# Reading a per-tile flag from a table instead of computing it in registers, in the expert stage of an attention and mixture-of-experts kernel

## The chip, the cores and the metric

The kernel runs on one core of a Trainium2 chip. The metric is the device time of one execution in microseconds (us), lower is better. Engines are named as the profile names them: PE (TensorE), ACT (ScalarE), DVE (VectorE), POOL (GpSimd), SP (SyncE, which here only issues DMAs). Each engine has a sequencer that reads its instruction stream; the profile marks what the sequencer does by itself (register arithmetic, branches, semaphore waits, register loads) with a q, as in ACTq.

## The reference

Three layers follow each other: windowed attention with sink keys (4 x 8 heads, 768 positions, head size 64), a mixture of experts over 3072 tokens, and a dense layer pair.

```python
def _moe_ref(x, w_skip, w_gate, w1, w2):            # x: 3072 x 512, 8 experts, F = 1024
    out = x.copy()
    do_compute = (x @ w_skip) > 0                     # the other tokens pass through
    xc = x[do_compute]
    e_idx = np.argmax(xc @ w_gate, axis=1)            # one expert for each token
    for e in range(8):
        h = np.maximum(xc[e_idx == e] @ w1[e], 0.0)
        y[e_idx == e] = gate_w[e_idx == e, None] * (h @ w2[e])
    out[do_compute] = xc + y
    return out

def _moe2_ref(x, w_in, w_out):                        # 512 -> 2048 -> 512
    r = np.maximum(x @ w_in, 0.0)
    return (r * r) @ w_out
```

## The kernel before, in words

The three layers run one after the other; the change touches the second, the expert stage, which takes the span's part from about 195 to 391 us. Tokens have been sorted by expert into rows of `routed`. The stage walks over tiles of 128 tokens, numbered n = 0, 1, 2 ..., and every expert e owns the tiles from `first` to `end`. How many an expert has is known only while the kernel runs: DVE computes it into the SBUF row `table`, and each engine reads `first` and `end` of an expert into registers with two `value_load` calls (lines 381 and 382). In this data there are 15 tiles: expert 0 has n = 0 to 2, experts 1 to 4 have two each (3 and 4, 5 and 6, 7 and 8, 9 and 10), experts 5 and 6 have one each (11 and 12), expert 7 has 13 and 14. The bodies for experts 0 and 1 are written out; experts 2 to 7 run in a hardware loop (line 373) whose body holds two experts, and inside each body a loop over n runs the tile's code.

Matrix products are made of an upper and a lower part of each operand for accuracy. While PE works on expert e with one pair of weight buffers, the next expert's weights are split into the other pair: SP loads them as 8 chunks of 512 KB into `w_raw`, ACT copies each chunk to `w_hi` (1.04 us or so), DVE subtracts to `w_lo` (1.22 us), and then SP may load the chunk of the expert after that into the same place. The eight chunks are two groups, the head (4 chunks, before the tile's own work) and the tail (4 chunks, in its middle). This is done in an expert's first tile. In later tiles of the same expert the same code makes one chunk of each group again, so that all counts of semaphores stay simple. The number that tells these apart is the flag `later`: 0 in the first tile of an expert, 1 in later ones. ACT and DVE need it in every tile (number of chunks, first chunk, values to wait for), ACT needs it a second time for the tile before, and SP needs it once per expert, for the expert's last tile.

Before, the flag is register arithmetic, `min(max(n - first, 0), 1)`:

```python
ahead, more, flag = (eng.alloc_register(...) for _ in range(3))
eng.reg_alu(ahead, n, first, op=ALU.subtract)
eng.reg_alu(more, ahead, 0, op=ALU.max)
eng.reg_alu(flag, more, 1, op=ALU.min)
```

Within a tile, ACT's order is: head chunks (line 748), `relu_b` for half 0 of the hidden layer (tile `h_b`, line 710), `hb_hi` (714), `relu_b` for half 1, `xb_hi` of the next tile (673), `hb_hi` again, tail chunks (748). PE's order is: layer 1 (line 975) for half 0 and the first half of half 1, then `turn_h(0)`, a transpose of ACT's `h_b` (line 983), the rest of layer 1, the transpose of the next tile's tokens (967), and layer 2 (994). DVE's order is: head chunks (1430), `hb_lo` (1385), `xb_lo` (1306), `hb_lo`, tail chunks, and the output row `y_row` and `y_id` (1392, 1394). All engines work through their streams in order.

Of the kernel before, what the change touches and what calls it, by code (L numbers as in the profile page):

```python
# [22 lines left out]
F32, F32R, BF16, I32 = mybir.dt.float32, mybir.dt.float32r, mybir.dt.bfloat16, mybir.dt.int32  # L23
# [17 lines left out]
MAX_TILES = N // P + 2 * E  # L41
# [3 lines left out]
UNIT = 8  # L45
HEAD = 4
# [27 lines left out]
def build(nc, n_sink, window, qT, kT, v, v_sink, w_route, weights, out):  # L74
# [10 lines left out]
    with ctx:  # L85
        def sem(name):
            return ctx.enter_context(nc.semaphore(name))
# [33 lines left out]
        def sbr(name, shape, dt):  # L121
            return sb(name, shape, dt, small, "right")

        pad_row = sbr("pad_row", [P, ROW], F32)
        table = sbr("table", [1, 3 * E], I32)
        rows = sbr("rows", [1, MAX_TILES + 2], I32)
        least = sbr("least", [1, E], F32)
        tile_no = sbr("tile_no", [1, MAX_TILES + 2, E], I32)
        row_of = sbr("row_of", [1, 4, MAX_TILES + 2, E], F32)
# [82 lines left out]
        s_xstore = [sem(f"s_xstore{n}") for n in range(XR)]  # L212
        s_scatter = [sem(f"s_scatter{n}") for n in range(XR)]
        s_tchain, s_table, s_padrow = sem("s_tchain"), sem("s_table"), sem("s_padrow")
        s_rchain, s_rows = sem("s_rchain"), sem("s_rows")

        s_w0 = [sem(f"s_w0{n}") for n in range(UNIT)]
        s_whead, s_wtail = sem("s_whead"), sem("s_wtail")
# [128 lines left out]
            first, size = ((0, HEAD), (HEAD, UNIT - HEAD))[k]  # L347
            return size - later * (size - 1), later * (size - 1) + first

        def is_later(eng, n, first):  # L350

            ahead, more, flag = (eng.alloc_register(f"later_{nc.next_id()}") for _ in range(3))
            eng.reg_alu(ahead, n, first, op=ALU.subtract)
            eng.reg_alu(more, ahead, 0, op=ALU.max)
            eng.reg_alu(flag, more, 1, op=ALU.min)
            return nc.s_assert_within(eng.snap(flag), 0, 1, skip_runtime_bounds_check_because="held to 0 and 1 above")

        def chunk_at(k, shift):

# [8 lines left out]
        def each_expert(eng, body):  # L368

            for e in range(2):  # L370
                first, end = expert_tiles(eng, e)
                body(e, e, 0 if e == 0 else first, end)
            with eng.Fori(1, E // 2) as m:
                for slot in range(2):
                    e = m * 2 + slot
                    first, end = expert_tiles(eng, e)
                    body(e, slot, first, end)
# [9 lines left out]
        def _(eng):  # L387
# [85 lines left out]
            def expert(e, slot, first, end):  # L473

                made = parts_ahead(e, first)
                for f in range(UNIT):
                    if f == HEAD - 1 or f == UNIT - 1:
                        last = parts_ahead(e + 1, end) - (UNIT - HEAD if f < HEAD else 0)
                        if f < HEAD:
                            last = is_later(eng, end - 1, first) * (UNIT - HEAD - 1) + last  # L480
                        eng.wait_ge(s_wlo, last)
                        close(eng)
                    else:
                        eng.wait_ge(s_wlo, made + f + 1)
                        close(eng)
                    load_chunk(e + 2, f)
# [137 lines left out]
        def _(eng):  # L624
# [105 lines left out]

            def tile(e, n, slot, first):

                later = is_later(eng, n, first)

                def chunks(k):
                    size, shift = group(k, later)
                    made = parts_ahead(e, n) + (later * (UNIT - 2) if k == 0 else later * (UNIT - HEAD - 1) + HEAD)
                    eng.wait_ge(s_whi, made)
                    close(eng)

                    before_is_later = is_later(eng, n, first + 1) if k == 0 else 0
                    lower = parts_ahead(e, n) + later * (UNIT - 2)
                    eng.wait_ge(s_wlo, lower if k == 1 else lower - (UNIT - HEAD) + before_is_later * (UNIT - HEAD - 1))
                    close(eng)
                    chunk_loaded(e + 1, k * HEAD)
                    with eng.Fori(0, size) as c:
                        f = bass.ds(chunk_at(c, shift), 1)
                        eng.activation(w_hi[1 - slot][:, f, :], w_raw[:, f, :], ACT.Copy).then_inc(s_whi, 1)  # L748

                chunks(0)  # L750
                relu_b(n, 0)
                h_upper(n, 0)
                relu_b(n, 1)
                x_upper(n + 1)
                h_upper(n, 1)

                eng.wait_ge(s_by, n + 1)
                chunks(1)
# [6 lines left out]
            gate(TILES - 1)  # L765
            first_tile()
            eng.wait_ge(s_table, 1)
            each_expert(eng, expert)


# [366 lines left out]
        def _(eng):  # L1137
# [266 lines left out]
            chain(eng.scalar_tensor_tensor(out=row_of[:, 3, :, :], in0=row_of[:, 0, :, :], scalar=0.0, in1=row_of[:, 2, :, :], op0=ALU.is_ge, op1=ALU.mult))  # L1404
            chain.end()
            eng.tensor_reduce(rows[:, :], row_of[:, 3, :, :], AX.X, ALU.max).then_inc(s_rows, 1)
            h_lower(0, 0)
            h_lower(0, 1)
            for f in range(0, 3):
# [4 lines left out]
            for f in range(4, UNIT):  # L1414
                lower_chunk(eng, 1, f, (s_whi, UNIT + f + 1), s_wlo)
            eng.wait_ge(s_table, 1)

            def tile(e, n, slot, first):
                later = is_later(eng, n, first)

                def chunks(k):
                    size, shift = group(k, later)
# [15 lines left out]

            def expert(e, slot, first, end):
                with eng.Fori(1 if isinstance(e, int) and e == 0 else first, end) as n:  # L1440
                    tile(e, n, slot, first)
            each_expert(eng, expert)


# [86 lines left out]
```

## Time and profile before

| | |
|---|---|
| median of three runs | 961.18 us (961.46, 955.9, 961.18) |
| the profiled execution's own time | 961.46 us |
| span of the profile, first to last instruction | 960.0 us |
| mean granted TensorE clock | 0.989 of full speed |
| PE busy | 928.3 us, 97% of the span |
| DVE, ACT busy | 456.0 and 419.8 us |
| PE waits inside the expert stage that are laid to ACT's `h_b` | 3.9 us, 3 times |

The span and the time differ by 1.46 us in the profiled execution, for what lies around the first and last instruction. The busy time of ACT and DVE counts only their data instructions; what a sequencer does by itself does not count, so an engine that shows as idle can have a busy sequencer.

### The profile page before, as it was taken

The page shows a single profiled execution, that of the slowest core. Times are in us where ns is not written, and L with a number is a line of the kernel's source. Part 1 is how long each engine was busy: PE and PEld are TensorE (multiplying, and loading weights), DVE is VectorE, ACT ScalarE, POOL GpSimd, SP SyncE. Part 2 cuts the span into 40 slices and gives each one's busy share as a digit, 9 for nine tenths or more (in the row PEclk, how much of TensorE's full clock was granted, in tenths as well). Part 3 has the DMA queues.
Part 4 walks back from the last instruction along what each step waited for, and adds up shares of the span by engine and source line. Part 5 has one row for each costly group of instructions (what it writes and reads, how often), then busy time and mean ns, then how long its engine had stood idle before and what let it go on. Part 6 is the DMA issues. An engine that isn't in the chain of part 4 may idle for free.

```text
span 960.0 us, 17066 instructions
## 1 busy us (share of the span) xinstructions
PE 928.3 (97%) x5240; PEld 743.9 (77%) x5241; DVE 456.0 (47%) x1392; ACT 419.8 (44%) x969; POOL 82.4 (9%) x148
## 2 busy tenths in 40 slices
PE   7999999989999999599999999999999999999998
PEld 5778777767888877488888888888888888888886
DVE  5787899785767778343232223222322222222223
ACT  6888999745666677243122123112321222122122
POOL 3112111223111111000000000000000000000000
PEclk9999999989999999799999999999999999999999
DMA  5456774376666687600020002000200020002001
GB/s 179 167 169 207 226 233 149 121 278 215 240 238 223 224 314 256 240 4 1 0 71 19 1 1 87 0 0 0 87 0 0 0 87 0 0 0 87 0 0 44
DMA packets 40291, 100.04 MB, mean 104 GB/s; under 512 B 5821, under 2 KB 5949, under 8 KB 40240
## 3 DMA queue, kind: packets, MB, share of 16 engines
q1 hardware_dynamic: 33936, 83.33, 25.5%
q0 software_dynamic: 6160, 16.02, 4.8%
q8 instruction: 25, 0.41, 0.2%
q14 instruction: 26, 0.21, 0.1%
q10 hardware_dynamic: 144, 0.07, 0.0%
HBM read 78.25 MB, written 25.56 MB: 108 GB/s over the span
## 4 chain that ended last, share of the span: by engine, by line
PE 90%; DVE 3%; DMA 2%; issue 2%; ACT 1%; DVEq 0%; ACTq 0%; SPq 0%; POOLq 0%; POOL 0%
PE bank L1090 28%; PE bank L1104 28%; PE bank L994 7%; PE bank L975 7%; PE bank L834 5%; PE bank L889 4%; PE bank L862 4%; PE bank L900 1%; PE bank L983 1%; DMA w_raw<-in_weights 1%; PE bank L1071 1%; PE bank L914 1%; PE bank L882 1%; PE bank L967 1%; ACT prob L640 0%
## 5 line engine op out<-in xcount | busy, mean ns | idle before, releaser
L1455 DVE TENSOR_TENSOR g<-relu_c 128x512 f32<-128x512 f32 x96 | 66.5, 692 | 364.9 <-ACT relu_c L780 364.8
L780 ACT ACTIVATE relu_c<-bank 128x512 f32<-128x512 f32 x96 | 57.4, 598 | 388.6 <-PE bank L1090 388.6
L1090 PE MATMUL bank<-x_hi,w_lo 128*128 128x512 f32 x384 | 152.6, 398 | 0.8 <-DVE x_lo L1448 0.8
L1104 PE MATMUL bank<-w_hi,g_lo 128*128 128x512 f32 x384 | 153.1, 399 | 0.0
L1090 PE MATMUL bank<-x_lo,w_hi 128*128 128x512 f32 x384 | 152.8, 398 | 0.0
L1090 PE MATMUL bank<-x_hi,w_hi 128*128 128x512 f32 x384 | 152.8, 398 | 0.0
L1104 PE MATMUL bank<-w_hi,g_hi 128*128 128x512 f32 x384 | 152.0, 396 | 0.0
L1104 PE MATMUL bank<-w_lo,g_hi 128*128 128x512 f32 x384 | 151.8, 395 | 0.0
L640 ACT ACTIVATE prob<-score,neg_max 128x264 f32<-128x264 f32 (+1 forms) x192 | 94.0, 496 | 16.6 <-DVE neg_max L1164 16.6
L1430 DVE TENSOR_TENSOR w_lo<-w_raw,w_hi x70 | 82.0, 1221 | 21.2 <-ACT w_hi L748 11.1
L1090 PEld LDWEIGHTS bank<-x_hi,w_lo 128*128 128x128 f32 x384 | 72.6, 189 | 19.0 <-DVE x_lo L1448 1.2
L1090 PEld LDWEIGHTS bank<-x_lo,w_hi 128*128 128x128 f32 x384 | 72.7, 189 | 17.9
L1090 PEld LDWEIGHTS bank<-x_hi,w_hi 128*128 128x128 f32 x384 | 72.8, 190 | 17.5
L1104 PEld LDWEIGHTS bank<-w_hi,g_hi 128*128 128x128 f32 x384 | 72.3, 188 | 17.6
L1104 PEld LDWEIGHTS bank<-w_lo,g_hi 128*128 128x128 f32 x384 | 72.4, 188 | 16.9
L1104 PEld LDWEIGHTS bank<-w_hi,g_lo 128*128 128x128 f32 x384 | 72.1, 188 | 16.8
L1164 DVE CUSTOM_DVE_ANT_0 score<-bank,masks 128x264 f32<-128x264 f32 (+1 forms) x192 | 74.5, 403 | 16.0 <-PE bank L834 7.3
L748 ACT ACTIVATE w_hi<-w_raw x70 | 69.5, 1051 | 18.5 <-DVE w_lo L1430 9.5
L1459 DVE TENSOR_TENSOR g_lo<-g,g_hi 128x512 fp32r<-128x512 f32 x96 | 65.8, 686 | 7.7 <-ACT g_hi L786 7.7
L786 ACT ACTIVATE g_hi<-g 128x512 fp32r<-128x512 f32 x96 | 59.9, 624 | 9.9 <-PE bank L1104 9.9
L834 PE MATMUL bank<-k_in,q_in 64*128 64x264 f32 (+1 forms) x384 | 55.9, 409 | 5.7 <-DMA k_in<-in_kT 5.6
L862 PE MATMUL bank<-ident,prob 128*128 128x128 f32 x352 | 56.1, 283 | 3.6 <-ACT probT L653 2.9
(141 smaller groups left out, 1285.3 us busy)
## 6 DMA issues: line engine op xcount, KB each, us to landing
w_raw<-in_weights SPq DMA_DIRECT2D x80, 512.0 KB, 5.1
x_c<-x_rows SPq DMA_DIRECT2D x28, 256.0 KB, 3.6
k_in<-in_kT SPq DMA_DIRECT2D x24, 264.0 KB
q_in<-in_qT SPq DMA_DIRECT2D x24, 256.0 KB, 3.1
v_in<-in_v SPq DMA_DIRECT2D x24, 256.0 KB
x_rows<-x_row SPq DMA_DIRECT2D x24, 256.0 KB
out<-w_raw SPq DMA_DIRECT2D x12, 512.0 KB, 2.8
x_res<-routed POOLq DMA_DIRECT2D x16, 260.0 KB, 4.5
```

The source lines that it names most:

```text
L640: eng.activation(prob[:, i % 2, h, 0:width(i)], score[:, i % 2, h, 0:width(i)], ACT.Exp, bias=neg_max[:, i % 2, h:h + 1], scale=-1.0, accu ...
L748: eng.activation(w_hi[1 - slot][:, f, :], w_raw[:, f, :], ACT.Copy).then_inc(s_whi, 1)
L834: eng.matmul(score_ps[n % SCORE_BANKS][:, 0:width(i)], q_in[rows, i % 3, h // 2, :], keys, start=True, stop=True).then_inc(s_score, 1)
L862: ins = eng.transpose(to[:, u * P:(u + 1) * P], prob[:, i % 2, 2 * k + half, at * KB + NS:(at + 1) * KB], ident[:, :])
L975: ins = eng.matmul(h_ps[half][:, :], x[:, c, :], w[:, c, cols], start=(c == 0 and k == 0), stop=(c == DC - 1 and k == 2))
L994: ins = eng.matmul(y_ps[:, :], h[:, c // 4, at], w[:, DC + c // 2, cols], start=(c == 0 and k == 0), stop=(c == FC - 1 and k == 2))
L1090: ins = eng.matmul(hc_ps[f % 2][:, :], w[f // UNIT][:, f % UNIT, wcols], x[:, c, :], start=(c == 0 and n == 0), stop=(c == DC - 1 and n == 2))
L1104: ins = eng.matmul(yc_ps[s][:, :], gg[:, f % 2, s * P:(s + 1) * P], w[f // UNIT][:, f % UNIT, DM:CH], start=(f == 0 and n == 0), stop=(f = ...
L1164: eng.tensor_tensor_reduce(score[:, i % 2, h, 0:width(i)], score_ps[n % SCORE_BANKS][:, 0:width(i)], masks[:, mask_kind(i), 0:len(blocks(i ...
L1430: eng.tensor_tensor(w_lo[1 - slot][:, f, :], w_raw[:, f, :], w_hi[1 - slot][:, f, :].bitcast(F32), ALU.subtract).then_inc(s_wlo, 1)
L1455: eng.tensor_tensor(g[:, f % 2, :], relu_c[:, f % 2, :], relu_c[:, f % 2, :], ALU.mult).then_inc(s_cg, 1)
L1459: eng.tensor_tensor(g_lo[:, f % 2, :], g[:, f % 2, :], g_hi[:, f % 2, :].bitcast(F32), ALU.subtract).then_inc(s_cglo, 1)
```

## The change

The flag of every tile is computed once, by DVE, right behind the row numbers `rows`: a compare of `row_of[:, 0]` (tile number less the first tile of each expert) with zero, and a minimum over the experts, into the new SBUF row `later_tile`, with a semaphore `s_later`. `is_later` then is a `value_load` from that row at index n. ACT and DVE wait for `s_later` once, before their loops; SP before its first use of it in experts 0 and 1. For the tile before, ACT reads index n - 1. That value is 1 at the first tile of an expert if the expert before had more than one tile, where the arithmetic gave 0, so the number that ACT waits for on `s_wlo` there is higher by 3.

```diff
+        later_tile = sbr("later_tile", [1, MAX_TILES + 2], I32)
...
-        def is_later(eng, n, first):
-
-            ahead, more, flag = (eng.alloc_register(f"later_{nc.next_id()}") for _ in range(3))
-            eng.reg_alu(ahead, n, first, op=ALU.subtract)
-            eng.reg_alu(more, ahead, 0, op=ALU.max)
-            eng.reg_alu(flag, more, 1, op=ALU.min)
-            return nc.s_assert_within(eng.snap(flag), 0, 1, skip_runtime_bounds_check_because="held to 0 and 1 above")
+        def is_later(eng, n):
+
+            return eng.value_load(later_tile[0:1, bass.ds(n, 1)], min_val=0, max_val=1)
...
                         if f < HEAD:
-                            last = is_later(eng, end - 1, first) * (UNIT - HEAD - 1) + last
+                            if isinstance(e, int):
+                                eng.wait_ge(s_later, 1)
+                            last = is_later(eng, end - 1) * (UNIT - HEAD - 1) + last
...
-                later = is_later(eng, n, first)
+                later = is_later(eng, n)
...
-                    before_is_later = is_later(eng, n, first + 1) if k == 0 else 0
+                    before_is_later = is_later(eng, nc.s_assert_within(n - 1, 0, MAX_TILES, skip_runtime_bounds_check_because="tile 0 is written out")) if k == 0 else 0
...
             eng.tensor_reduce(rows[:, :], row_of[:, 3, :, :], AX.X, ALU.max).then_inc(s_rows, 1)
+            eng.tensor_scalar(row_of[:, 1, :, :], row_of[:, 0, :, :], 0.0, None, ALU.not_equal).then_inc(s_rchain, 1)
+            eng.wait_ge(s_rchain, 6)
+            eng.tensor_reduce(later_tile[:, :], row_of[:, 1, :, :], AX.X, ALU.min).then_inc(s_later, 1)
```

The first place is ACT at the start of a tile, in the looped body for experts 3, 5 and 7, from the entry of the loop over n to the first head chunk. Before (an ISA row is one fused group of register operations, or an assertion behind a load):

```order
L738 ISA
L353 ISA [waits s_whi]
L743 REGISTER_ALU
L310 ISA [waits s_wlo]
L746 UNCONDITIONAL_BRANCH [waits s_whead]
L746 ISA
L748 ACTIVATE w_hi<-w_raw 128x1024
```

The same place after the change:

```order
L353 TENSOR_LOAD later_tile
L353 ISA x2
L737 ISA
L353 ISA [waits s_whi]
L353 TENSOR_LOAD later_tile
L353 ISA x2
L742 ISA
L311 ISA [waits s_wlo]
L745 UNCONDITIONAL_BRANCH [waits s_whead]
L745 ISA
L747 ACTIVATE w_hi<-w_raw 128x1024
```

Two loads, each with its two ISA rows, stand between the loop's entry and the first chunk; the second is behind the wait for `s_whi`, ACT's own last chunk.

The second place is DVE at the start of a tile, in the same body. Before:

```order
L1440 UNCONDITIONAL_BRANCH
L1440 ISA
L1424 ISA
L1426 UNCONDITIONAL_BRANCH [waits s_wlo]
L1426 ISA
L1430 ISA [waits s_whi]
L1430 REGISTER_ALU
L1430 TENSOR_TENSOR w_lo<-w_raw,w_hi 128x1024
```

After:

```order
L1445 UNCONDITIONAL_BRANCH
L1445 ISA
L353 TENSOR_LOAD later_tile
L353 ISA x2
L1429 ISA
L1431 UNCONDITIONAL_BRANCH [waits s_wlo]
L1431 ISA
L1435 ISA [waits s_whi]
L1435 REGISTER_ALU
L1435 TENSOR_TENSOR w_lo<-w_raw,w_hi 128x1024
```

One load comes in ahead of DVE's first chunk of each tile. Once in the kernel, two DVE instructions come in ahead of `hb_lo` of tile 0:

```order
L1406 TENSOR_REDUCE rows<-row_of 1x42 [waits s_rchain]
L1407 TENSOR_SCALAR row_of<-row_of 1x336
L1409 TENSOR_REDUCE later_tile<-row_of 1x42 [waits s_rchain]
L1385 TENSOR_TENSOR hb_lo<-bank,hb_hi 128x512 [waits s_bhhi] x2
L339 TENSOR_TENSOR w_lo<-w_raw,w_hi 128x1024 [waits s_whi] x3
L1306 TENSOR_TENSOR xb_lo<-bank,xb_hi 128x512 [waits s_bxhi]
```

The new instructions are rows two and three; everything below them on DVE's stream stands two places later than before.

## Rows read from the trace of the kernel before

**Rows 1.** The page: busy time of each engine.

```profile
PE 928.3 (97%) x5240; PEld 743.9 (77%) x5241; DVE 456.0 (47%) x1392; ACT 419.8 (44%) x969; POOL 82.4 (9%) x148
```

**Rows 2.** Busy time by stretch: PE, PEld, DVE, ACT, POOL, granted clock, DMA share, GB/s.

```profile
213.00:391.30 178.30, 173.94 (x840) 141.12 (x840) 124.56 (x146) 111.15 (x143) 34.82 (x48) 1.00 0.71 250
```

**Rows 3.** Waits of PE, 195 to 392 us: total us, times, longest.

```profile
PE bank L983 <- ACT h_b L710: 3.9, 3, 1.8
...
PE bank L975 <- DVE xb_lo L1306: 0.5, 1, 0.5
```

**Rows 4.** Timeline of PE: start, us, instruction [idle before, releaser]; transposes of `h_b`.

```profile
217.77 0.44 PE L983 MATMUL bank<-ident,h_b 128*128 128x128 f32 x2 [0.42 <-ACT h_b L710]
...
316.54 0.60 PE L983 MATMUL bank<-ident,h_b 128*128 128x128 f32 x4
...
341.21 0.60 PE L983 MATMUL bank<-ident,h_b 128*128 128x128 f32 x4
...
355.86 0.66 PE L983 MATMUL bank<-ident,h_b 128*128 128x128 f32 x4 [1.73 <-ACT h_b L710]
```

**Rows 5.** Timeline of ACT at first tiles of an expert.

```profile
315.50 0.57 ACT L710 ACTIVATE h_b<-bank 128x512 f32<-128x512 f32 x1
...
333.23 1.06 ACT L748 ACTIVATE w_hi<-w_raw  x1
336.13 3.90 ACT L748 ACTIVATE w_hi<-w_raw  x4 [1.85 <-DVE w_lo L1430]
340.05 0.60 ACT L710 ACTIVATE h_b<-bank 128x512 f32<-128x512 f32 x1
...
351.42 3.90 ACT L748 ACTIVATE w_hi<-w_raw  x4 [1.92 <-DMA w_raw<-in_weights]
355.23 0.57 ACT L710 ACTIVATE h_b<-bank 128x512 f32<-128x512 f32 x1
```

**Rows 6.** Waits of ACT, 213 to 392 us: total us, times, longest.

```profile
ACT h_b L710 <- PE bank L975: 20.0, 20, 3.9
ACT w_hi L748 <- DVE w_lo L1430: 9.5, 5, 2.1
```

**Rows 7.** Chain that ended last, ACT's and DVE's sequencers around 348 and 351 us.

```profile
347.79 0.28 ACTq L381
...
348.44 0.28 ACTq L382
...
351.08 0.31 DVEq L381
...
351.73 0.07 DVEq L382
```

**Rows 8.** Single lines on the sequencers: duration ns min/median/max, first and last start.

```profile
L353 ACTq FUSED_REGOPS  x14: 175/178/181, 215.6 to 378.7; - x14
L761 ACTq FUSED_REGOPS  x14: 172/192/198, 212.5 to 376.6; - x14
L1440 DVEq FUSED_REGOPS  x14: 207/242/253, 218.0 to 379.7; - x14
L381 DVEq TENSOR_LOAD <-table x8: 314/322/1092, 215.5 to 365.4; - x8
```

**Rows 9.** Timeline of DVE: rows for the row numbers, `xb_lo`, and a head group.

```profile
206.77 0.49 DVE L1406 TENSOR_REDUCE rows<-row_of 1x42 int32<-1x336 f32 x1
...
211.79 0.67 DVE L1306 TENSOR_TENSOR xb_lo<-bank,xb_hi 128x512 fp32r<-128x512 f32 x1
...
340.61 2.36 DVE L1430 TENSOR_TENSOR w_lo<-w_raw,w_hi  x2 [2.29 <-issue]
```

**Rows 10.** Timeline of SP: the first reload of a head chunk at tile 11.

```profile
342.08 0.33 SPq L415 DMA_DIRECT2D w_raw<-in_weights  x1
```

**Rows 11.** Busy time by stretch, as in Rows 2, around tiles 11 and 12.

```profile
340.00:342.00 2.00, 2.00 (x13) 1.67 (x12) 1.39 (x2) 0.79 (x3) 0.81 (x2) 1.00 0.39 110
...
358.00:360.00 2.00, 2.00 (x14) 1.70 (x12) 1.63 (x3) 1.29 (x3) 0.55 (x1) 1.00 0.89 320
```

More of the change, by code:

```diff
@@ L214, in build @@
         s_tchain, s_table, s_padrow = sem("s_tchain"), sem("s_table"), sem("s_padrow")
-        s_rchain, s_rows = sem("s_rchain"), sem("s_rows")
+        s_rchain, s_rows, s_later = sem("s_rchain"), sem("s_rows"), sem("s_later")
         s_w0 = [sem(f"s_w0{n}") for n in range(UNIT)]
@@ L767, in _ @@
             eng.wait_ge(s_table, 1)
+            eng.wait_ge(s_later, 1)
             each_expert(eng, expert)
@@ L1416, in _, with tile @@
             eng.wait_ge(s_table, 1)
-            def tile(e, n, slot, first):
-                later = is_later(eng, n, first)
+            eng.wait_ge(s_later, 1)
+            def tile(e, n, slot):
+                later = is_later(eng, n)
                 def chunks(k):
@@ L1440, in expert @@
                 with eng.Fori(1 if isinstance(e, int) and e == 0 else first, end) as n:
-                    tile(e, n, slot, first)
+                    tile(e, n, slot)
             each_expert(eng, expert)
```

## The prediction

> **What bounds the kernel now.** I read the page first: PE is busy for 97% of the span [rows 1], so a change to register code on other engines costs something only where PE waits for one of them. The change touches the expert stage alone, so the next views are that stage's. From the start of tile 1 to the end of tile 14 PE is busy for 173.94 of 178.30 us at a granted clock of 1.00, which is the 2.4 GHz level [rows 2]. Its waits from 195 us on are few, and the largest kind is the transpose of `h_b` waiting for ACT: three times, 3.9 us in all, the longest 1.8 us [rows 3]. They stand in tiles 1, 12 and 13: 0.42 us at 217.77, 1.73 us at 355.86, and the 1.8 us of the third [rows 3, 4]. These three tiles are already late, and what makes ACT or its weights later there is paid in full.
>
> The first tiles of experts 1 to 5 (n = 3, 5, 7, 9 and 11) show no wait, so the question is how much room they have. At n = 11 ACT makes the four head chunks from 336.13 and runs straight into `h_b` at 340.05, which ends at 340.65; PE takes it at 341.21 [rows 4, 5]. Where PE was waiting, it began 0.06 us after `h_b` ended (355.23 + 0.57 against 355.86 [rows 4, 5]). So the room at n = 11 is 341.21 - 340.65 - 0.06 = 0.50 us. At n = 9 it is 316.54 - 316.07 - 0.06 = 0.41 us [rows 4, 5]; n = 3, 5 and 7 repeat n = 11's pattern with 0.51 us each. **This is the figure the case turns on: a delay of ACT's head group under half a microsecond is free, and all above it is PE's.**
>
> What starts that head group is the next thing to read. At n = 11 the chunk before it starts at 333.23 and the group at 336.13, 2.90 us later, of which ACT's data path is idle for 1.85 us. The view names DVE's `w_lo` as releaser [rows 5], but the count that ACT waits for there had been reached a tile earlier; the gap comes at all five of these tiles, 9.5 us in all, 2.1 at most [rows 6], because it is the sequencer's own work: the end of one loop, two loads from `table`, the flag, the waits, the next loop. One chunk of 1.06 us does not cover that. Instructions added to the sequencer there are therefore exposed.
>
> **Price of one load.** The loads of lines 381 and 382 are of the same form as the new ones: one number from an SBUF row, its bounds check and assertion. On ACT the first starts at 347.79 and the second, with its address in front of it, at 348.44: 0.65 us each with the address [rows 7]. On DVE the load with its check takes 351.73 - 351.08 = 0.65 us [rows 7], and some 0.11 us more with its address: 0.76 us.
>
> **ACT, per tile.** Two loads come in, 2 x 0.65 = 1.30 us. The second flag's fused group of 0.18 us (L353) goes, and the group at the loop's entry that held the first flag (0.19 us, L761) becomes the first load's address, which is in the 0.65 already [rows 8]. Net x = 1.30 - 0.18 - 0.19 = 0.93, say **0.9 us**. From below x is bounded by two bare loads of 0.28 us less the two groups, 0.2 us, and from above by nothing saved: 1.3 us [rows 7, 8]. I take 0.9 because it is built of the same instructions on the same sequencer. By tile:
> - n = 3, 5, 7: 0.9 - 0.51 = 0.39 us each, 1.2 us. n = 9: 0.9 - 0.41 = 0.5 us.
> - n = 1: the sequencer runs ahead of four queued chunks, so the first load is hidden behind them; the second stands behind the wait for ACT's last chunk. It adds 0.65 - 0.18 = 0.5 us to an `h_b` for which PE already waits (0.42 us [rows 4]): 0.5 us.
> - n = 2 and second tiles (4, 6, 8, 10, 14): only one chunk is made, and `h_b` then waits for PE; these are among the 20 waits of 20.0 us in all, 1.0 us each on average [rows 6]. The first load hides behind the tail chunks, the second's 0.5 us fits into that wait. Nothing.
> - n = 12, 13: ACT waits for the DMA of the weights (1.92 us at 351.42 [rows 5]), and the loads fit into that wait. What moves the DMA is DVE.
>
> **DVE, per tile.** One load comes in, 0.76 us, and the fused group at the loop's entry (0.24 us, L1440 [rows 8]) shrinks to the address: net some **0.5 us**, between 0.1 (the bare load of 0.32 less that group) and 0.8 us. In two-tile experts DVE has room: nothing on PE waits for it but the 0.5 us at the stage's start [rows 3]. It matters where SP's reloads feed the next tile, n = 11 to 13. There the head group starts when the sequencer is ready (340.61, 2.29 us idle, released by issue [rows 9]). SP issues the first reload at 342.08 [rows 10], and at that time the DMA engines are at 39% [rows 11], so a reload issued 0.5 us later lands 0.5 us later; this weight's arrival ends ACT's wait at 351.42 and so PE's at 355.86. I charge 0.5 us at n = 12, which takes in n = 11's own 0.4. At n = 13 DVE is later by its own load once more, but by then the DMA engines are at 89% and more [rows 11] and the chunks queue behind each other, so I charge nothing there, at most 0.5 us. Together **0.5 us, at most 1.2.**
>
> **DVE, once.** Two instructions of the size of the reduce at 206.77, 0.49 us each with 336 elements [rows 9], come in: 1.0 us. `xb_lo` for tile 1 then ends at 213.5 instead of 212.46 [rows 9], and PE, which comes to it at 213.00, waits up to 0.5 us. It is not lost a second time: PE waits for `h_b` at 217.77 in the same tile, and by n = 1's line above that wait ends at 218.27 whether PE comes early or late. Cover: that wait, 0.42 + 0.5 us. Without it the cost would be 0.5 us. POOL's `s_rows` comes before the new pair and does not move.
>
> **SP and the raised count.** SP's load is done before it waits for DVE's last chunk. In two-tile experts that wait lasts most of a tile. At n = 11 and 12 the load stands between the third and the fourth reload, 1.2 us apart [rows 9], and may make the fourth 0.2 us late, behind a full queue: nothing. The wait for `s_wlo` that is higher by 3 asks for DVE's head chunk of the tile before, which is done long before ACT comes there: nothing.
>
> **Sum.** 0.5 (n = 1) + 1.2 (n = 3, 5, 7) + 0.5 (n = 9) + 0.5 (n = 11 to 13) = **2.7 us**. The profiled execution took 961.46 us, so it would be 964.2; the median of the runs shown is 0.28 us below that, so I predict 963.9, rounded to **964.0 us**, 0.3% slower. The last layer, from 403 us on, reads no flag and has the same instructions.
>
> **The rivals.**
> - *All hidden, 961.5 us.* The sequencer reads a load while the engine works on queued instructions, as at 347.79, amid tile 11's tail chunks [rows 7]. If that held everywhere, only n = 1's half microsecond or less would be left. Against it: at n = 3 to 11 one chunk of 1.06 us covers a path of 2.90 us [rows 5]. For it: x could be near its lower end, 0.2 us, and under 0.5 us five of the terms are zero. The Trainium skill (Advanced Engine Details and Errata, Sequencer and Instruction Queues with Engine Queue Depths) says that other engine instructions are queued while a control instruction executes and gives ScalarE and VectorE a queue of 8; by that alone all loads would be hidden. The trace agrees with it at 347.79 and not at 336.13, where the queue had run dry.
> - *Slower on the other side of 1%, 974 us.* The first load on DVE took 1.09 us, against a median of 0.32 [rows 8]. If reading a row that another engine wrote cost every load 0.8 us more, x would be 2.5 us: five tiles with 2.0 each, n = 1 with 1.3, and 1.3 for n = 11 to 13, 12.6 us in all. It decides from x above 2.0. Against it: seven of eight loads were near the median, and the slow one was the first behind a new wait.
> - *Moved code, 968.5 us.* ACT's program grows by 26 instructions and DVE's by 15, so code in the looped body sits elsewhere in memory. If each of the three passes through it then had to fetch instructions again, at 1.5 us each (a gap of the size ACT's sequencer already hides or shows at 336.13 [rows 5]), 4.5 us would come on top. Nothing in the trace speaks for it. The Trainium skill (the same page, ISA Cache) gives a cache of two lines of 256 instructions outside TensorE; no row here shows a refetch.
> - *The flags save time, 959 us.* The removed register work is 0.37 us per ACT tile; even free loads would give back at most that at n = 1 and some tenths at 12 and 13, under 1.5 us. No path to 1%.
>
> **How the numbers follow.** Likeliest (962.5 to 966) 0.64; all hidden (961 to 962.5) 0.18; moved code or loads somewhat dearer than priced (966 to 970.5) 0.12; over 970.8 us 0.04; saving 0.02. A measurement of this kernel tells about 1% (9.6 us) from no change: faster by more than that 0.01, within it 0.95, slower 0.04. The costs alone would give 961 to 968.5. One of the three runs shown is 5.3 us below the others, and a median could fall there, which takes the low end to 957.5. Range 957.5 to 968.5.
>
> **What would show it.** In the changed profile: ACT's head group starts 3.8 instead of 2.90 us after the chunk before it at n = 3 to 11; waits of PE for `h_b` of about 0.4 us appear there, five new ones beside the three old; the wait at tile 1 grows to 0.9 us; loads of line 353 take 0.28 us on ACT and 0.32 on DVE. The prediction is wrong if those head groups start no later, or if loads are far from 0.3 us, or if the difference lies outside 213 to 391 us.

## The result, and the profile after

The kernel after takes 963.03 us (median of 15 runs, 960.11 to 968.17), the kernel before, run beside it, 958.64 us (15 runs, 954.69 to 961.76). The ratio is 1.0058 with a 95% interval of 1.0038 to 1.0079, so the change costs 5.6 us, between 3.6 and 7.6: slower, and within the 1% that the prediction called no change. (The ratio is worked out from the single times and is not the quotient of the two medians, which lie 4.4 us apart; the means lie 5.6 apart. The same holds for the ratios below.) Its profiled execution took 963.35 us. All ratios are of fast runs; one run of the kernel before, of 29 in the first set below, took 1824.7 us and is in none of them.

The page after (PE's busy time is 1.3 us longer than in [rows 1]), the windows, and the waits of PE from 195 to 392 us:

```profile
PE 929.6 (97%) x5240; PEld 742.6 (77%) x5241; DVE 456.8 (47%) x1394; ACT 418.9 (44%) x969; POOL 82.2 (9%) x148
```

```profile
213.00:356.00 143.00, 140.53 (x666) 111.45 (x664) 95.04 (x112) 86.09 (x112) 27.88 (x38) 1.00 0.68 236
356.00:361.00 5.00, 4.42 (x17) 3.65 (x18) 3.62 (x4) 1.91 (x5) 0.00 (x0) 0.66 0.96 343
```

```profile
PE bank L983 <- ACT h_b L709: 4.2, 4, 2.0
PE bank L967 <- DMA x_raw<-routed: 1.2, 1, 1.2
PE bank L975 <- DVE xb_lo L1306: 0.8, 1, 0.8
```

Two things stand out against [rows 2, 3]. PE's waits for `h_b` have hardly grown (4.2 us in 4 waits, before 3.9 in 3), although five new ones were forecast. And in the second window the granted clock is 0.66, where before it was 1.00.

The delay on ACT is there, to the tenth. ACT's timeline after, tile 11, which answers to 333.23 to 340.05 in [rows 5], and the load itself:

```profile
333.09 1.06 ACT L747 ACTIVATE w_hi<-w_raw  x1
336.88 3.90 ACT L747 ACTIVATE w_hi<-w_raw  x4 [2.73 <-issue]
340.69 0.57 ACT L709 ACTIVATE h_b<-bank 128x512 f32<-128x512 f32 x1
```

```profile
L353 ACTq TENSOR_LOAD <-later_tile x28: 273/278/640, 208.8 to 380.9; - x28
...
L353 DVEq TENSOR_LOAD <-later_tile x14: 298/313/808, 214.6 to 381.9; - x14
```

The head group starts 3.79 us after the chunk before it, instead of 2.90. But PE is not ready for `h_b` when it was. The transposes of `h_b` at n = 3, 4, 9, 11 and 12 (`turn_h(0)`), as in [rows 4]:

```profile
240.03 0.66 PE L983 MATMUL bank<-ident,h_b 128*128 128x128 f32 x4
...
252.63 0.60 PE L983 MATMUL bank<-ident,h_b 128*128 128x128 f32 x4
...
316.11 0.66 PE L983 MATMUL bank<-ident,h_b 128*128 128x128 f32 x4 [0.27 <-ACT h_b L709]
...
341.32 0.66 PE L983 MATMUL bank<-ident,h_b 128*128 128x128 f32 x4
...
356.58 1.04 PE L983 MATMUL bank<-ident,h_b 128*128 128x128 f32 x4 [1.99 <-ACT h_b L709]
...
361.42 0.60 PE L983 MATMUL bank<-ident,h_b 128*128 128x128 f32 x4
```

The last row is `turn_h(1)` of n = 12. In the kernel before it is this row, behind the `turn_h(0)` at 355.86 in [rows 4]:

```profile
359.10 0.60 PE L983 MATMUL bank<-ident,h_b 128*128 128x128 f32 x4
```

From n = 3 to n = 4, where nothing is waited for, PE takes 252.63 - 240.03 = 12.60 us. Before it took 12.32. PE's program is the same, so its matmuls themselves must follow each other more slowly. The starts of layer 1's matmuls show it. (The distance from one start to the next is called the pitch below.) Ahead of `turn_h(0)` stand 18 of them; tile 6 in the kernel before:

```profile
275.40 0.39 PE L975 MATMUL bank<-w_lo,xb_hi 128*128 128x512 f32 x1
...
279.26 0.39 PE L975 MATMUL bank<-w_hi,xb_hi 128*128 128x512 f32 x1
279.49 0.38 PE L983 MATMUL bank<-ident,h_b 128*128 128x128 f32 x2
```

and after:

```profile
273.72 0.39 PE L975 MATMUL bank<-w_lo,xb_hi 128*128 128x512 f32 x1
...
277.68 0.40 PE L975 MATMUL bank<-w_hi,xb_hi 128*128 128x512 f32 x1
277.92 0.60 PE L983 MATMUL bank<-ident,h_b 128*128 128x128 f32 x4
```

(279.49 - 275.40) / 18 = 227 ns from start to start, against (277.92 - 273.72) / 18 = 233 ns. Before, some half of each tile ran at 227 ns and the rest, behind the transposes, at 231 to 236; after, all of it runs at 233. The timeline's durations hardly show this (0.39 and 0.40), and no wait does; starts do. So do mean durations of many like instructions, if one compares them closely: the matmuls `bank<-w_hi,xb_lo` from 213 to 345 us take 390 ns on average before and 395 after. The last layer ran at 233.6 ns in both.

So three things had to be explained: the slower pitch, the loads, and tile 12, where `turn_h(1)` came 4.84 us behind `turn_h(0)` instead of 3.24.

The two profiled executions differ by only 1.9 us in span (961.9 and 960.0). From `turn_h(0)` of tile 0 to that of tile 14 the one after takes 185.79 us, the one before 179.87: 5.92 more. But the stretch ahead of it is 3.66 us shorter (199.12 against 202.78 us) and the one behind it 0.37. The new loads have no part in the stretch ahead: the first starts at 208.8 us. From 195 to 213 us the granted clock was 0.83 before and 0.96 after.

### The profile page after: what moved, and what is told of

Same layout as the page of the kernel before. It is cut to its first block, busy times and chain, and to the rows that moved or that the text cites. A ratio compares the mean times of both kernels' runs of the same rounds, so it can differ in the third digit from the quotient of the medians.

```text
span 961.9 us, 17222 instructions
## 1 busy us (share of the span) xinstructions
PE 929.6 (97%) x5240; PEld 742.6 (77%) x5241; DVE 456.8 (47%) x1394; ACT 418.9 (44%) x969; POOL 82.2 (9%) x148
## 4 chain that ended last, share of the span: by engine, by line
PE 89%; issue 3%; DMA 2%; ACT 2%; DVE 2%; ACTq 1%; DVEq 0%; SPq 0%; POOLq 0%; POOL 0%
PE bank L1090 28%; PE bank L1104 28%; PE bank L994 7%; PE bank L975 6%; PE bank L834 5%; PE bank L889 4%; PE bank L862 4%; PE bank L983 1%; PE bank L900 1%; PE bank L1071 1%; PE bank L914 1%; PE bank L882 1%; PE bank L967 1%; DMA w_raw<-in_weights 1%; ACT w_hi L747 1%
## 5 line engine op out<-in xcount | busy, mean ns | idle before, releaser
L747 ACT ACTIVATE w_hi<-w_raw x70 | 69.5, 1050 | 27.4 <-issue 15.6
```

## The experiments

### First set: where the slower pitch comes from

The new row `later_tile` stands in the middle of a group of SBUF tiles that are laid out downwards. Each tile declared behind it moves down by 192 bytes, `xb_hi`, `xb_lo`, `h_b`, `hb_hi` and `hb_lo` among them, from a multiple of 128 bytes to 64 past one. The first kernel has the move alone:

```diff
         rows = sbr("rows", [1, MAX_TILES + 2], I32)
+        unused = sbr("unused", [1, MAX_TILES + 2], I32)
```

> The kernel before, with nothing changed but an unused row of 168 bytes declared where the change declares later_tile. No instruction is added; the tiles declared behind it (xb_hi, xb_lo, h_b, hb_hi, hb_lo, y_row) lie 192 bytes lower, so that their start is no longer a multiple of 128 bytes. Theory A (the place of TensorE's stationary operands sets the pitch of its matmuls): the matmuls of 512 columns in the expert stage follow each other at 233 ns as after the change, not at 227 to 232, and the time is 3 to 3.5 us over before. Theory B (the slower pitch comes with the new loads or the moved code of ACT and DVE): pitch as before, difference 0. Theory C (the pitch is a matter of the single execution): it follows neither.

Measured: ratio 1.0029 (1.0011 to 1.0047), 2.8 us slower, from a row that nothing reads. Tile 6 in its trace:

```profile
273.20 0.39 PE L976 MATMUL bank<-w_lo,xb_hi 128*128 128x512 f32 x1
...
277.17 0.40 PE L976 MATMUL bank<-w_hi,xb_hi 128*128 128x512 f32 x1
277.41 0.60 PE L984 MATMUL bank<-ident,h_b 128*128 128x128 f32 x4
```

(277.41 - 273.20) / 18 = 234 ns. From n = 2 to n = 11 this trace loses 1.83 us against before, 0.20 in each tile, with no wait added. Theory A holds, and B and C fall. Its 3 to 3.5 us were a little high, but inside the interval of 1.1 to 4.5. The edit moves every tile declared behind it, those of ACT and DVE too; which of them matter is a question for the last set.

The second kernel has the change, with the row where it moves nothing:

```diff
-        later_tile = sbr("later_tile", [1, MAX_TILES + 2], I32)
...
         y_id = sbr("y_id", [P, 1], I32)
+        later_tile = sbr("later_tile", [1, MAX_TILES + 2], I32)
```

> The whole change, with later_tile declared last of its group, so that no other tile moves. Theory A: the pitch is that of before, ACT's head groups still start 3.8 us after the chunk before them, so PE now waits for h_b some 0.3 us at n = 3, 5, 7 and 11 and 0.6 us at n = 9, and n = 12 costs 0.6 us: about 2.5 us over before, less than the 5.6 us of the change. Theory B: 5 to 6 us over before and a pitch of 233 ns.

Measured: 1.0019 (1.0005 to 1.0033), 1.8 us over before (0.5 to 3.2), where 2.5 were expected. The pitch is 227 ns again, and now the waits that the prediction foresaw are there. ACT's and PE's timelines at n = 9:

```profile
307.11 1.06 ACT L747 ACTIVATE w_hi<-w_raw  x1
311.27 3.90 ACT L747 ACTIVATE w_hi<-w_raw  x4 [3.10 <-issue]
315.08 0.57 ACT L709 ACTIVATE h_b<-bank 128x512 f32<-128x512 f32 x1
```

```profile
315.70 0.66 PE L983 MATMUL bank<-ident,h_b 128*128 128x128 f32 x4 [0.48 <-ACT h_b L709]
```

`h_b` ends at 315.65 and PE takes it 0.05 us later. The intervals from one `turn_h(0)` to the next at n = 3, 5, 7, 9 and 11 are 12.65, 12.70, 12.60, 12.94 and 12.58 us, where before they were 12.36 each. At n = 12 the interval is 15.67 instead of 14.64 (0.6 more was expected), and at n = 13, where the granted clock fell as in the kernel after, 15.72 instead of 14.38.

The third keeps the row in place and adds 64 bytes, for a move of 256:

```diff
         later_tile = sbr("later_tile", [1, MAX_TILES + 2], I32)
+        unused = sbr("unused", [1, 16], I32)
```

> The whole change, with 64 unused bytes behind later_tile, so that the tiles behind lie 256 bytes lower and again begin at a multiple of 128 bytes. Theory A with 128 bytes as the step: pitch and time as with later_tile declared last, about 2.5 us over before. Theory A with another step, or some neighbour that matters: 233 ns and 5 to 6 us over before. Theory B: 5 to 6 us.

Measured: 1.0028 (1.0012 to 1.0044), 2.7 us over before, with the pitch of before (227.9 ns over layer 1 from 240 to 345 us, against 228.1 before and 233.0 after). So it is the position against 128 bytes, not the move, that counts. Its intervals at n = 3 to 11 repeat those of the second kernel to 0.03 us. The times of these two and of the kernel with the move alone can't be told from each other (1.8, 2.7 and 2.8 us, each known to 1.3 to 1.7); it is the pitches and the intervals that tell the causes apart.

If that is so elsewhere too, the last layer of the kernel before has something to give: `x_hi`, `x_lo`, `g_hi` and `g_lo` begin 96 bytes past a multiple of 128. The expectation calls all four moving operands, that is, operands whose 512 columns are streamed past a stationary one of 128x128. That is right for `x_hi` and `x_lo` (line 1090). In the layer's other half (line 1104) `g_hi` and `g_lo` are the stationary operands, as `xb_hi` is in line 975, and the weights stream; these lie at multiples of 128 in all kernels here.

```diff
+        unused = sb("unused", [P, 24], F32, side="right")
         x_c = sb("x_c", [P, 4, DM], F32, side="right")
```

> The kernel before, with 96 unused bytes ahead of x_c in the last layer's group, so that x_hi, x_lo, g_hi and g_lo begin at multiples of 128 bytes (they begin 96 bytes past one). They are the moving operands of the last layer, whose matmuls follow each other at 233.5 ns on average over some 2300 of them. Theory A, if it holds for moving operands too: the pitch there falls to 227 to 230 ns and the time by 8 to 15 us. If only stationary operands matter, or under theories B and C: no difference.

Measured: 943.13 us against 957.94, ratio 0.9837 (0.9815 to 0.9859), **15.6 us faster** with 96 unused bytes and nothing else. One block of the last layer, from its transposes of `x_c` to the next block's, in the kernel before:

```profile
579.69 1.04 PE L1071 MATMUL bank<-ident,x_c 128*128 128x128 f32 x8
...
671.15 1.04 PE L1071 MATMUL bank<-ident,x_c 128*128 128x128 f32 x8
```

and here:

```profile
569.71 1.04 PE L1072 MATMUL bank<-ident,x_c 128*128 128x128 f32 x8
...
658.57 1.04 PE L1072 MATMUL bank<-ident,x_c 128*128 128x128 f32 x8
```

91.46 us against 88.86: 2.60 us for each of six blocks, 15.6 us. (The medians lie 14.8 apart.) The pitch is 226.7 ns in the half with `x` and 226.9 in the half with `g` (226 or 227 in nearly all of over 2100 gaps), before 233.6 in both. Mean durations fall with it, from 396 to 389 ns for `bank<-x_hi,w_hi`.

### Second set: whose loads cost what

From here on the row is declared last in the kernels with one engine's loads, so that nothing moves. ACT alone reads from the table:

```diff
-                            last = is_later(eng, end - 1) * (UNIT - HEAD - 1) + last
+                            last = is_later_by_arithmetic(eng, end - 1, first) * (UNIT - HEAD - 1) + last
...
-            def tile(e, n, slot):
-                later = is_later(eng, n)
+            def tile(e, n, slot, first):
+                later = is_later_by_arithmetic(eng, n, first)
```

> The table is computed as in the change and later_tile is declared last, so that no tile moves; ACT alone reads its flags from the table, DVE and SP keep their register arithmetic. Theory A (ACT's two loads make its head group 0.8 to 0.9 us late, of which PE's room swallows some 0.5): turn_h(0) at n = 3, 5, 7, 9 and 11 comes 0.3, 0.3, 0.25, 0.6 and 0.2 us late, 1.7 us together, and the time is 1.5 to 2 us over before, with nothing lost at n = 12. Rival D (the loss at n = 12, 0.9 to 1.0 us with later_tile declared last, is ACT's too, through the chunk that SP may reload only when ACT and DVE have made it): 1 us more, of it at n = 12.

Measured: 1.0029 (1.0012 to 1.0046), 2.8 us over before. The intervals at n = 3, 5, 7, 9 and 11 are longer by 0.29, 0.31, 0.24, 0.57 and 0.22 us, 1.63 together; the second tiles take 12.38 instead of 12.32, another 0.25 for four. At n = 12 the interval is 14.54, before 14.64: nothing is lost there, and rival D falls as far as one trace can tell. The time is over the expected 1.5 to 2 us, which the interval (1.1 to 4.4) still holds; the trace has 1.1 us more at n = 1 (16.12 instead of 14.99), which the expectation left out.

DVE alone reads from the table (ACT's and SP's flags go back to arithmetic in the same way):

> As with ACT alone, but here DVE alone reads its flag from the table; ACT and SP keep the arithmetic. Theory A (DVE's later head group at n = 11 makes SP's reloads later, and those the weights of n = 12): no loss at n = 3 to 11, 0.5 to 1.0 us at n = 12 and nothing after it, if the clock holds. Rival D: nothing at n = 12 either, difference 0. If PE's idle time before turn_h(0) at n = 12 passes the 1.8 us of before and the granted clock falls there, as in the run with later_tile last (2.6 us idle), 1.2 to 1.6 us come on top.

Measured: 1.0006 (0.9990 to 1.0022): no difference that can be told. Nothing at n = 3 to 11; at n = 12 the interval is 15.75 instead of 14.64. PE's timeline and the windows behind it:

```profile
353.77 0.70 PE L988 MATMUL bank<-ident,h_b 128*128 128x128 f32 x4 [2.33 <-ACT h_b L715]
```

```profile
353.00:355.00 2.00, 1.23 (x6) 1.13 (x7) 2.00 (x3) 1.21 (x3) 0.00 (x0) 0.81 1.03 360
355.00:357.00 2.00, 2.00 (x6) 1.41 (x6) 1.26 (x2) 0.11 (x1) 0.00 (x0) 0.50 0.99 291
357.00:359.00 2.00, 2.00 (x14) 1.77 (x12) 0.49 (x1) 1.20 (x2) 0.40 (x1) 0.83 0.92 338
```

Here too the granted clock falls to 0.50, the 1.2 GHz level, right behind PE's wait. It costs 1.6 us between the two transposes, of which 0.8 come back at n = 13, where PE waits for weights anyhow: the interval there is 15.19, 0.8 over before.

Then all tiles of all three layers at multiples of 128 bytes, without the change and with it (the edit is shortened, the line in brackets stands for several):

```diff
         def sb(name, shape, dt, stack=ctx, side="left"):
+            size = (bytes of one partition, rounded up to 32)
+            spare = -size % 128
+            if side == "right" and spare:
+                stack.enter_context(nc.sbuf_tensor(f"spare_{name}", [P, spare // 4], F32, side=side))
```

> The kernel before with every SBUF tile of all three layers begun at a multiple of 128 bytes, by unused bytes between them. Theory A (place of TensorE's operands): the last layer's 15 us are gained as with its own operands aligned. What is left in the expert stage, 233 ns for half of each tile, comes either from the tiles that were still off (x_raw 32 bytes past, turned by TensorE in each tile), then those fall to 227 ns as well and another 1.5 us is gained, or from something else, then nothing more is gained there. The attention stage may gain 0 to 5 us. Forecast 940 us, 18 us under before.

Measured: 943.96 us, 0.9846 (0.9821 to 0.9870), the same as with the last layer's operands alone, and 4 us above the forecast of 940. The expert stage keeps its mixed pitch (228.2 ns for layer 1, as before), so the slower half of each tile is not due to `x_raw`'s position, and the attention stage gains nothing that shows. This execution lost some 0.6 us at n = 3 and again at n = 4, with no wait, and 1.5 us at n = 12; nothing explains the first two, and no other trace has them.

> The whole change on the kernel with every tile at a multiple of 128 bytes. The pitch is then that of its neighbour without the change, so the difference of the two is the price of the loads alone: 2 to 2.5 us by theory A (waits at n = 3 to 12), 5 to 6 us if the change's slower pitch had another cause than the tiles' places.

Measured: 946.87 us, 0.9876 (0.9852 to 0.9900) of before, 2.9 us more than its neighbour without the change. That is an estimate of the price of the loads with the positions equal (expected: 2 to 2.5), and a rough one: the two kernels ran 6 and 5 times, and their intervals overlap. In the traces the intervals of n = 3, 5, 7, 9 and 11 are 12.67, 12.69, 12.60, 12.96 and 12.60, as in the other kernels with ACT's loads, but because of what the neighbour's execution lost, the whole stage takes the same in both (183.14 and 183.18 us from tile 0 to tile 14).

### Third set: the price of a load, and how far the pitch reaches

ACT with one load instead of two (the second flag by arithmetic), and with four (two more loads of the same row, whose values go unused):

```diff
-                    before_is_later = is_later(eng, nc.s_assert_within(n - 1, ...)) if k == 0 else 0
+                    before_is_later = is_later_by_arithmetic(eng, n, first + 1) if k == 0 else 0
```

```diff
                     before_is_later = is_later(eng, nc.s_assert_within(n - 1, ...)) if k == 0 else 0
+                    if k == 0:
+                        is_later(eng, n)
+                        is_later(eng, n)
```

> ACT reads only its first flag from the table; its second (for the tile before), and the flags of DVE and SP, stay register arithmetic; later_tile is declared last. Theory A (a load costs the sequencer 0.6 us, and the room before turn_h(0) is 0.4 to 0.5 us): ACT's head group is 0.45 us late, which the room just covers, so no new wait at n = 3 to 11, or one under 0.1 us, and the time is that of before (0 to 0.5 us over). Rival L (what costs is not the loads' length but that the table is computed and read at all): 1.5 to 2.5 us over before, as with two loads.

> ACT alone reads flags from the table, and behind the second load of each tile two more loads of the same row are made whose values go unused. Theory A: the group is another 1.25 us late, which PE pays in full at n = 3, 5, 7, 9 and 11 (1.5 us late each, 1.8 at n = 9, instead of 0.2 to 0.6) and at n = 1, and 0.2 to 0.3 us at n = 4, 6, 8 and 10, where the room was 0.5 us and the group was already 0.5 us late: 9 to 11 us over before. Rival H (most of a load is hidden, and the loss of the two loads is a matter of their place): under 5 us over before.

Measured: one load 1.0014 (0.9998 to 1.0030), not told from before; four loads 1.0162 (1.0142 to 1.0183), 15.5 us over before. ACT at n = 9 with one load, then ACT and PE with four:

```profile
305.03 1.06 ACT L753 ACTIVATE w_hi<-w_raw  x1
308.76 3.90 ACT L753 ACTIVATE w_hi<-w_raw  x4 [2.67 <-issue]
312.57 0.58 ACT L715 ACTIVATE h_b<-bank 128x512 f32<-128x512 f32 x1
```

```profile
312.10 1.06 ACT L756 ACTIVATE w_hi<-w_raw  x1
317.32 3.90 ACT L756 ACTIVATE w_hi<-w_raw  x4 [4.16 <-issue]
321.12 0.58 ACT L715 ACTIVATE h_b<-bank 128x512 f32<-128x512 f32 x1
```

```profile
321.76 0.66 PE L992 MATMUL bank<-ident,h_b 128*128 128x128 f32 x4 [1.53 <-ACT h_b L715]
```

From the chunk before to the group, with no, one, two and four of ACT's loads:

| n | none | one | two | four |
|---|---|---|---|---|
| 5 | 2.97 | 3.38 | 3.88 | 4.95 |
| 9 | 3.14 | 3.73 | 4.14 | 5.22 |
| 11 | 2.91 | 3.32 | 3.79 | 4.94 |
| interval of PE at n = 11 | 12.36 | 12.32 | 12.58 | 13.77 |

(us; none is the kernel before, two the kernel with ACT's loads alone.) Each load is paid on the sequencer, 0.4 to 0.6 us where it replaces a fused group and 0.5 to 0.6 where it replaces nothing. PE sees none of the first one (at n = 9 its interval grows by 0.16), a quarter of a microsecond of the second, and all of the next two. Rival H falls. Of rival L (reading the table costs as such) the trace leaves next to nothing at n = 3 to 11; the time alone, 1.4 us over before (-0.2 to 2.9), would not exclude it. Four loads cost more than the 9 to 11 us expected: by the trace n = 3, 5, 7, 9 and 11 take 7.5 us more than before and n = 1 another 1.9, n = 12 and 13 add 1.8, and n = 14, behind a fall of the granted clock (0.57 from 379 to 383 us), 1.6. That makes 12.8 us; where the rest of the 15.5 goes the trace doesn't show.

The last layer's operands at 64 bytes past a multiple of 128:

```diff
+        unused = sb("unused", [P, 8], F32, side="right")
         x_c = sb("x_c", [P, 4, DM], F32, side="right")
```

> The kernel before with 32 unused bytes ahead of x_c, so that x_hi, x_lo, g_hi and g_lo begin 64 bytes past a multiple of 128 instead of 96. If a multiple of 64 is enough for a moving operand: a pitch of 227 ns in the last layer and 14 to 15 us under before. If it takes 128, as the stationary operands of the expert stage seem to: 233.5 ns, no difference.

Measured: 0.9976 (0.9964 to 0.9989), 2.3 us faster: neither of the two. The block of the last layer takes 91.08 us (91.46 before, 88.86 at a multiple of 128):

```profile
574.66 1.03 PE L1072 MATMUL bank<-ident,x_c 128*128 128x128 f32 x8
...
665.74 1.03 PE L1072 MATMUL bank<-ident,x_c 128*128 128x128 f32 x8
```

So the position acts by degrees: 0.38 us of 2.60 are had at 64 past. Nearly all of it is in the half that streams `x` (231.9 ns, from 233.6); the half with `g` stationary is at 233.3.

Stationary operands of layer 2 alone out of place:

```diff
         h_b = sbr("h_b", [P, 2, F // 2], F32)
+        unused = sbr("unused", [P, 16], F32)
         hb_hi = sbr("hb_hi", [P, 2, F // 2], F32R)
```

> The kernel before with 64 unused bytes between h_b and hb_hi, so that hb_hi and hb_lo begin 64 bytes past a multiple of 128 while xb_hi and xb_lo stay at one. If the place of each matmul's own stationary operand sets its pitch: layer 2 (from hb) at 233 ns throughout, layer 1 (from xb) at 227 in the stretch where it was so before. If one misplaced operand sets TensorE off for a longer while: both at 233.

One execution, 960.73 us, which tells nothing by itself. In the trace the matmuls from `hb_lo` follow at 229.3 ns (227.4 before) and those from `xb_lo` at 228.1 (227.6), and a tile takes 12.35 us, as before. Neither reading is right: with `hb` alone out of place almost nothing is lost, with `x_raw`, `xb`, `h_b`, `hb` and the tiles around them all moved 0.2 us per tile. Which of them it takes was not tried further, and so it isn't shown that the stationary operands are the ones that count in the expert stage.

## Why the prediction was right, and where it wasn't

The forecast was 964.0 us, the measurement is 963.03. That they agree to 1 us is luck: two errors of some 3 us offset each other. **The base**: the sum was made against one profiled execution of 961.46 us, while the kernel before had a median of 957.6 to 958.6 in each of the four sets of runs, some 3 us lower. That execution lost its time ahead of the change's stage: tile 0's `turn_h(0)` comes at 202.78 us, in eleven of the other thirteen traces at 199.1 to 200.3. **The sum**: 2.7 us, where 5.6 (3.6 to 7.6) were measured. About half of the difference has a cause that no step named.

- *"The last layer ... has the same instructions", and PE's matmuls taken as unchanged: the step that failed, by omission.* The diff's first line, a new SBUF row, was read as free. It moved TensorE's operands, among others, and costs 2.8 us alone (1.1 to 4.5). A change of PE's pace with no instruction changed was in none of the rivals; "moved code" came nearest in form, and had the wrong cause.
- *Room of 0.50, 0.41 and 0.51 us, ACT's x = 0.9 us: right.* The group came 0.89 us later, and with the positions equal PE paid 0.29, 0.31, 0.24, 0.57 and 0.22 us at n = 3, 5, 7, 9 and 11, for 0.39, 0.39, 0.39, 0.5 and part of 0.5. That is 1.63 us over the five, for some 2. The difference is on ACT: `h_b` begins 3.81 us behind the start of the head group (340.69 - 336.88 in the kernel after), where it was 3.92 (340.05 - 336.13 in [rows 5]), and ends 0.14 sooner after it. In the kernel after itself the profile shows a wait at n = 9 alone, where five were forecast, because a slower PE needs `h_b` 0.25 us later. What is left of them is under what a profile marks as idle: at n = 11, too, PE begins 0.06 us after `h_b` ends (341.32 against 340.69 + 0.57), with no time idle. The two costs overlap: from n = 2 to 11 the move alone loses 1.83 us, the loads alone 1.95, both 2.86.
- *Second tiles at nothing:* 0.06 us each in truth, 0.25 together. It is lost between `turn_h(0)` and `turn_h(1)` of the tile before (3.25 us behind a wait, 3.20 without one); why is open.
- *n = 1 at 0.5 us:* the interval there was 15.5 to 16.2 us with ACT's two loads, and 14.6 to 15.7 in kernels with before's flags, 14.99 in before's own trace. About 1 us rather than 0.5, and too scattered to size from single traces. The wait of PE there, forecast at 0.9 us, was 0.52 in the kernel after and 0.7 to 1.1 in the four kernels with both loads and no slower pitch.
- *DVE's two instructions, once, at nothing:* the wait for `xb_lo` that they were to bring is there (0.77 us, ahead of the 0.52 us for `h_b` in the same tile). Two kernels that compute the table and have at most one load on ACT take 15.17 and 15.19 us at n = 1, within the scatter of before's flags, so it is covered, as forecast.
- *DVE's 0.5 us at n = 11 to 13:* all five profiled kernels in which DVE loads its flag have 15.3 to 15.8 us at n = 12, before has 14.6. But three kernels with all of before's flags show 15.1 to 16.1 as well, and DVE's loads alone measure 0.6 us (-1.0 to 2.1). The term may be 0.5 to 1 us; it isn't shown.
- *Tile 13 at nothing, and the clock:* after's trace loses another 1.4 us between `turn_h(0)` of n = 12 and of n = 13, behind a wait of 1.99 us, at a granted clock of 0.66 from 356 to 361 us. That is a matter of the execution more than of the change: such a fall came in 6 of the 13 other kernels that were profiled (the one after among them), two of them without any load, and not in three whose PE waited 2.4 to 2.7 us at n = 12. With four loads it came behind n = 13 and not behind the wait of 3.0 us at n = 12. All six had a longer wait there than before's 1.73 and 1.8, so later weights may raise the odds; that is argued, not shown. In the kernel after it cost more than any single term of the sum, and the forecast had no term for it.
- *The rival "all hidden", with the Trainium skill's queue of 8 (Advanced Engine Details and Errata, Engine Queue Depths):* it falls at these places. The trace shows ACT's data path idle for 2.73 us ahead of the head group, so nothing is left in the queue to cover a load, and the table above shows each load in full.
- *SP, the raised count, free loads' gain:* nothing in any trace speaks of them, as forecast. Loads took 0.28 us on ACT and 0.31 on DVE, as forecast.

Sum of the parts, each timed: 2.8 (the move) + 1.8 to 2.9 (the loads: 1.8, 2.7 and 2.9 in three kernels) = 4.6 to 5.7 us, for 5.6 measured. That is no proof to the tenth: each part is known to 1.3 us at best, and by the traces they overlap by 0.9 us from n = 2 to 11, so that 3.7 to 4.8 would be due, which the measured interval of 3.6 to 7.6 holds.

## What to carry to other kernels

Ask of every line of a diff what it moves, not only what it executes: a declaration that shifts the operands of the bounding engine can cost as much as the code that it was made for, and lining them up can bring more than five times that. On the sequencers, a path between two pieces of work is worth timing end to end: its room is spent by fractions of a microsecond, and by the traces the first load was all but free where the second was not. When an engine's waits don't add up to the time lost, compare start-to-start distances, or mean durations in ns, of like instructions in both traces.

A forecast of a small difference needs a base from many runs: here one execution was 3 us off, as much as the sum itself.

The version to keep is the kernel before with 96 unused bytes ahead of `x_c`: 943.13 us, 1.6% under before and 2.1% under after (943.13 / 963.03, from different sets of runs).

## What the runs showed of the hardware

- **The position of operands in SBUF sets the pace of matmuls.** In the last layer 128x128 by 128x512 matmuls in this kernel's fp32 formats follow each other at 226.7 ns with the moving operand `x` at a multiple of 128 bytes, at 231.9 at 64 past and at 233.6 at 96 past: 3.0%. The half with `g` stationary goes with it: 226.9, 233.3 and 233.6. Both were moved together and the halves alternate, so what either does alone isn't shown. In the expert stage stationary operands and the tiles around them at 64 past held the pitch at 233 throughout, and `hb` alone at 64 past did almost nothing (229.3 ns instead of 227.4 for `hb_lo`). The Trainium skill (SBUF — State Buffer, Operand start alignment) asks for a multiple of the element size and says of its rule that it is "about legality, not speed"; the speed is what these runs show. What causes it is open, and so is whether tiles that only ACT and DVE read have a part in it.
- **A pitch can be lost for a while.** With all operands in place the expert stage still runs at 231 to 236 ns from the first transposes of `h_b` until some ten matmuls behind the last, and at 227 from there on. Why was not settled.
- **A register load from SBUF** costs ACT's sequencer 0.28 us bare and 0.5 to 0.6 with address, bounds check and assertion (0.53 to 0.58 each for the two added loads of the table above), in full where ACT's data path has run dry.
